# Delta-rule attention with two mixture layers on one core: the first group of linear systems on VectorE alone, P by partial sums, the second keys on ScalarE's queue

## What is computed

```
k_n = k / (|k| + 1e-6);  state = 0                       # 4 batches x 8 heads, 768 tokens, 48 features
for t: y_t   = q_t . state                               # with the state before the token
       state += beta_t * outer(k_n_t, v_t - state^T k_n_t)
x = y as 3072 tokens x 384
x = ((x@w1) * (x@w2)) @ w3 @ w_out                       # 384 -> 1024 -> 1024 -> 384
logits = x @ phi                                         # 32 slots
slots  = softmax(logits over tokens)^T @ x -> 8 experts of 4 slots: relu(s@e1)@e2
out    = softmax(logits over slots) @ slot_out
```

## Time and profile before

| | us |
|---|---|
| runs shown, lowest / median / highest | 546.17 / 548.49 / 549.38 |
| profiled execution: device time | 547.8 |
| profiled execution: span of the trace | 546.1 |
| PE busy | 495.9 (91%) |
| DVE / POOL / ACT busy | 249.7 / 207.8 / 139.0 |
| mean granted TensorE clock | 0.957 of full speed |

### The profile page before, as it was taken

One profiled execution on the slowest core, in us unless ns is written; L12 is line 12 of the kernel. 1 busy time (PEld: TensorE's weight loads), 2 busy tenths in 40 slices (PEclk: granted clock), 3 DMA queues, 4 the chain that ended last, 5 costly groups with the idle time before them and its releaser, 6 DMA issues.

```text
span 546.1 us, 24802 instructions
## 1 busy us (share of the span) xinstructions
PE 495.9 (91%) x11482; PEld 356.9 (65%) x11482; DVE 249.7 (46%) x537; ACT 139.0 (25%) x271; POOL 207.8 (38%) x386
## 2 busy tenths in 40 slices
PE   5797599979999999999899989999989999779974
PEld 5734457767777777777677867777767777324533
DVE  2699777255532554325462343633422421444424
ACT  0104212213222223222322223232212222104313
POOL 1077359850588006880048810488200000000000
PEclk9999589989999999999999999999999999689997
DMA  8996000440002500025000260000430607995938
GB/s 214 364 289 266 2 4 4 109 127 6 4 2 83 156 4 4 4 64 173 4 4 4 59 178 4 4 4 4 167 145 4 233 5 258 413 368 194 361 143 346
DMA packets 28439, 65.18 MB, mean 119 GB/s; under 512 B 1968, under 2 KB 15408, under 8 KB 28080
## 3 DMA queue, kind: packets, MB, share of 16 engines
q1 hardware_dynamic: 27888, 62.81, 34.2%
q10 hardware_dynamic: 448, 0.79, 0.6%
HBM read 58.87 MB, written 4.72 MB: 116 GB/s over the span
## 4 chain that ended last, share of the span: by engine, by line
PE 81%; DVE 9%; issue 4%; DMA 2%; ACT 1%; DVEq 0%
PE pB L1062 19%; PE pA L1062 18%; PE pD L1007 4%; PE pY L1017 4%; PE pK L989 4%; PE pK L967 3%; PE pT L1078 3%; PE pG L1078 3%; PE pY L974 2%; DVE prep_slab L673 2%; PE pD L1086 2%; DVE prep_slab L672 2%; PE pG L948 2%; PE pT L948 2%; PE pT L1028 2%
## 5 line engine op out<-in xcount | busy, mean ns | idle before, releaser
L428 POOL TENSOR_TENSOR prod_p<-prep_slab 128x84 f32<-128x84 f32 (+14 forms) x175 | 85.6, 489 | 49.3 <-DVE prep_slab L664 36.4
L429 POOL TENSOR_TENSOR prep_slab<-prep_slab,prod_p 128x84 f32<-128x84 f32 (+14 forms) x175 | 92.2, 527 | 13.7
L612 DVE TENSOR_TENSOR arena<-a_sb,pB 128x512 f32<-128x512 f32 x42 | 28.9, 688 | 142.7 <-PE pB L1062 142.5
L1062 PE MATMUL pB<-whi,xhi 128*128 128x512 f32 x138 | 59.6, 432 | 0.0
L1062 PE MATMUL pB<-whi,xlo 128*128 128x512 f32 x138 | 54.8, 397 | 0.4 <-issue 0.4
L1062 PE MATMUL pB<-wlo,xhi 128*128 128x512 f32 x138 | 54.5, 395 | 0.0
L1062 PE MATMUL pA<-whi,xhi 128*128 128x512 f32 x138 | 52.3, 434 | 0.0
L420 POOL TENSOR_SCALAR_AFFINE_SELECT prep_slab<-prep_slab 128x1024 f32<-128x1024 f32 x6 | 7.6, 1265 | 111.3 <-DVE sys_s L632 111.3
L1062 PE MATMUL pA<-whi,xlo 128*128 128x512 f32 x138 | 48.6, 402 | 0.0
L1062 PE MATMUL pA<-wlo,xhi 128*128 128x512 f32 x138 | 47.9, 400 | 0.8 <-issue 0.8
L471 ACT ACTIVATE a_sb<-pA 128x512 f32<-128x512 f32 x48 | 28.8, 600 | 68.8 <-PE pA L1062 61.0
(11 more groups left out here) (229 smaller groups left out, 844.3 us busy)
## 6 DMA issues: line engine op xcount, KB each, us to landing
late_w<-e_dram SPq DMA_DIRECT2D x8, 1536.0 KB, 9.1
arena<-kq_dram SPq DMA_DIRECT2D x44, 192.0 KB, 5.0
arena<-e_dram SPq DMA_DIRECT2D x5, 1536.0 KB, 11.7
arena<-kv_dram SPq DMA_DIRECT2D x16, 384.0 KB, 5.7
out_dram<-late_w SPq DMA_DIRECT2D x6, 768.0 KB, 5.3
arena<-w3t_dram SPq DMA_DIRECT2D x2, 2048.0 KB, 20.1
arena<-w_dram SPq DMA_DIRECT2D x1, 4096.0 KB, 14.1
late_w<-w_dram SPq DMA_DIRECT2D x2, 1536.0 KB, 19.7
```

Source lines behind the costliest of these rows:

```text
L428: link(nc.gpsimd.tensor_tensor(pv, a, x, ALU.mult))
L429: link(nc.gpsimd.tensor_tensor(dst, dst, pv, ALU.add))
L612: nc.vector.tensor_tensor(ab_tile(s, p)[:, half * HF:(half + 1) * HF], a_sb[:], pB[:], ALU.mult).then_inc(ab_done, 1)
L1062: last = mm((pA, pB)[w][:], lhs[:, c * 128:(c + 1) * 128], rhs[:, w, c, fc], start=(k == 0), stop=(k == 3 * KC - 1))
```

## The change

1. PE: `FILLERS` 80 -> 48.
2. Group 0 is solved by DVE alone, all columns in `X`, with no second copy in `At` and no mask by POOL: the mask comes with `first_keys`, which copies the Gram to `Gs` on DVE through `upto`. ACT copies the raw query-key part (`pt_raw`), and DVE masks it later in place (`first_pt`).
3. Step 0: R is values times norms (DVE, ahead of `scale`); `key_query_state` is left out; `y_step` goes ahead of `state_step` and starts the bank itself. In step 1 `up(0,0,0)` goes ahead of `key_query_state`, and the other parts change places.
4. P: the products of w_out and phi, and of wp and w3^T, go to separate 32-partition quadrants of a bank as partial sums; ACT copies them to `parts` and PE adds them by a product with `same`.
5. The second keys are issued from ACT's queue behind the copy of `wp`; kv of group 0 goes ahead of w1 on SP.
6. PE: after the Grams of group 1, 15 products of 128 x 512 (`AWAKE`), the one of k waiting for elimination step k of DVE, k = 15 to 29.
7. ACT: the Grams of group 1 are copied out before step 0, `w_high(0)` after them, `w_high(1)` in step 1.

```diff
-COL0_FIRST = 5
-FILLERS = 80
+FILLERS = 48
+AWAKE = range(15, 30)
 ...
-            reload_kq(1, 1)
+            load_kv(0, 0)
             sp.dma_start(w_raw[0], ...)
-            load_kv(0, 0)
             sp.dma_start(w_raw[1], ...)
-            sp.wait_ge(wp_ps, 1)
+            sp.wait_ge(part_ps, 2)
             load_kv(1, 1)
 ...  # POOL
+                if is_first(n):
+                    pool.wait_ge(x_link, 2)
+                    values(1, STEPS)
+                    return
 ...  # ACT
             for s in range(STEPS):
-                gram_out(0, s, first_gram[0][s])
+                act.wait_ge(gs_done, s + 1)
+                nc.scalar.activation(PT[0][:, s], <query-key part of the bank>, ACT.Copy).then_inc(pt_raw, 1)
+            part_out(0, 32 * KC)
+            part_out(1, 32 * KC)
             act.wait_ge(wp_ps, 1)
             nc.scalar.activation(wp_sb, pK[:, 0:FC * NS], ACT.Copy).then_inc(wp_done, 1)
-            pt_out(0)
-            w_high(0)
-            pt_out(1)
+            for i in range(H // 2):
+                for r in range(2):
+                    act.dma_start(*kq_piece(1, 1, i, r)).then_inc(kq_in[1][r], 16)
+            part_out(2, 128)
+            part_out(3, 128)
             act.wait_ge(p_ps, 1)
             nc.scalar.activation(P_sb, pY[:, 0:FC * NS], ACT.Copy).then_inc(p_done, 1)
-            w_high(1)
+            for s in range(STEPS):
+                gram_out(1, s, first_gram[1][s])
+            w_high(0)
 ...  # DVE
+            def first_keys(s, bank):
+                dve.wait_ge(gram_done, s + 1)
+                nc.vector.tensor_tensor(Gs[...s...], bank[... 0:C], upto[...], ALU.mult).then_inc(gs_done, 1)
 ...
-                for dst in (X, At) if is_first(n) else (X,):
-                    link(nc.vector.tensor_tensor(dst[:], At[:], ...
+                link(nc.vector.tensor_tensor(X[:], At[:], ...
 ...  # solve_first
-                    pv, a, x, dst = update(prod_d, At, k_, 0, min(k_, COL0_FIRST))
+                    pv, a, x, dst = update(prod_p, X, k_, 0, k_)
 ...
             solve_first()
+            r_rows(0, 0, 0, 0)
             scale(0)
             turn_back(0, 0)
                     if g == 0:
-                        r_rows(g, p, s, n)
+                        first_pt(0, 1)
                         for i in range(STEPS):
                             mask_pt(1, q, i, first_gram[1][i])
+                        first_pt(1, STEPS)
                         state(g)
                         set_up(1, q, k)
 ...  # PE
+            def add_parts(ps, rows_, sem_):
+                for c in range(FC):
+                    last = mm(ps[:, c * NS:(c + 1) * NS], parts[0:rows_, c * 128:(c + 1) * 128],
+                              same[0:rows_, 0:NS], start=True, stop=True)
+            for i in range(2):
                 for c in range(KC):
-                    last = mm(pK[:, g * NS:(g + 1) * NS], wot_raw[:, c, g * 128:...], phi_sb[:, c, :], ...)
+                    last = mm((pY, pK)[i][32 * c:32 * c + 32, :], phi_sb[:, c, :], wot_raw[:, c, i * HF:...], ...)
+            add_parts(pK, 32 * KC, wp_ps)
 ...
                 for c in range(FC):
-                    last = mm((pY, pK)[i][0:NS, :], wp_sb[:, c, :], w3t_raw[i][:, c, :], ...)
+                    g = c % 4
+                    last = mm((pY, pK)[i][32 * g:32 * g + 32, :], wp_sb[:, c, :], w3t_raw[i][:, c, :], ...)
+            add_parts(pY, 128, p_ps)
 ...
             for s in range(STEPS):
                 gram_products(1, s, first_gram[1][s])
+            for k_ in AWAKE:
+                pe.wait_ge(prep_link, X_LINK + 2 * k_)
+                mm(pK[:], ident[:], Macc[:, 0:HF], start=True, stop=True)
 ...
                     if g == 0:
                         solve_rows(g, p, s, n)
+                        y_step(g, p, s)
                         state_step(g, p, k, s, n)
-                        y_step(g, p, s)
                         x_turn(g)
                         continue
+                    if g == 1:
+                        up(t, 0, 0); key_query_state(g, p, k, s); up(t, 0, 1); solve_rows(g, p, s, n)
+                        up(t, 1, 0); state_step(...); ab_turn(...); y_step(g, p, s); up(t, 1, 1); x_turn(g)
+                        continue
```

More of the change, by code:

```diff
@@ L209, in delta_moe_kernel @@
         consts = sem("consts")
+        mask_in = sem("mask_in")
         diag_z = sem("diag_z")
@@ L422, in prep @@
                 pool.wait_ge(prep_link, prep_base(n) + X_LINK)
-                col0 = COL0_FIRST if is_first(n) else 0
-                for k_ in range(col0 + 1, C - 1):
-                    if not is_first(n) and k_ == VALUES_AT:
+                for k_ in range(1, C - 1):
+                    if k_ == VALUES_AT:
                         values(0, 1)
-                    pv, a, x, dst = update(prod_p, X, k_, col0, k_)
+                    pv, a, x, dst = update(prod_p, X, k_, 0, k_)
                     link(nc.gpsimd.tensor_tensor(pv, a, x, ALU.mult))
                     link(nc.gpsimd.tensor_tensor(dst, dst, pv, ALU.add))
-                if is_first(n):
-                    pool.wait_ge(x_link, 2)
-                    values(0, 1)
                 values(1, STEPS)
@@ L778, in _ @@
                                         ALU.add).then_inc(macc_done, 1)
-            for s in range(STEPS - 1):
-                mask_pt(0, 0, s, first_gram[0][s])
+            dve.wait_ge(macc_done, INIT_MACC)
+            nc.vector.tensor_tensor(upto[:], upper[:], same[:, 0:C], ALU.add).then_inc(mask_in, 1)
+            dve.wait_ge(mask_in, 1)
+            for s in range(STEPS):
+                first_keys(s, first_gram[0][s])
             set_up(0, 0, 0)
-            mask_pt(0, 0, STEPS - 1, first_gram[0][STEPS - 1])
             set_up_root(0)
@@ L954, in key_query_state @@
             def key_query_state(g, p, k, s):
-                if s == 0 and g > 0:
+                if s == 0:
                     for r in range(2):
@@ L1017, in y_step @@
                         last = mm(pY[o:o + 32, h * D:h * D + D], PT[p][q, s, h, :], Z[q, h, :],
-                                  start=False, stop=(h == H - 1), skip_group_check=True)
+                                  start=(g == 0 and h == 0), stop=(h == H - 1), skip_group_check=True)
                 last.then_inc(y_ps, 1)
@@ L1129, in _ @@
                     gram_products(0, s, first_gram[0][s], 2 * i, 2 * i + 2)
+            def add_parts(ps, rows_, sem_):
+                for c in range(FC):
+                    last = mm(ps[:, c * NS:(c + 1) * NS], parts[0:rows_, c * 128:(c + 1) * 128], same[0:rows_, 0:NS],
+                              start=True, stop=True)
+                last.then_inc(sem_, 1)
             pe.wait_ge(phi_in, 16)
             pe.wait_ge(wot_in, 16)
-            for g in range(FC):
+            for i in range(2):
                 for c in range(KC):
-                    last = mm(pK[:, g * NS:(g + 1) * NS], wot_raw[:, c, g * 128:(g + 1) * 128], phi_sb[:, c, :],
-                              start=(c == 0), stop=(c == KC - 1))
-            last.then_inc(wp_ps, 1)
+                    last = mm((pY, pK)[i][32 * c:32 * c + 32, :], phi_sb[:, c, :], wot_raw[:, c, i * HF:(i + 1) * HF],
+                              start=True, stop=True)
+                last.then_inc(part_ps, 1)
+            pe.wait_ge(macc_done, INIT_MACC)
+            pe.wait_ge(part_done, 2)
+            add_parts(pK, 32 * KC, wp_ps)
             pe.wait_ge(wp_done, 1)
@@ L1141, in _ @@
                 for c in range(FC):
-                    last = mm((pY, pK)[i][0:NS, :], wp_sb[:, c, :], w3t_raw[i][:, c, :], start=(c == 0),
-                              stop=(c == FC - 1))
-                last.then_inc(pt_ps, 1)
-            pe.wait_ge(pt_done, 2)
-            for c in range(FC):
-                last = nc.tensor.transpose(pY[:, c * NS:(c + 1) * NS], pt_sb[:, c * 128:(c + 1) * 128],
-                                           ident[0:NS, 0:NS])
-            last.then_inc(p_ps, 1)
+                    g = c % 4
+                    last = mm((pY, pK)[i][32 * g:32 * g + 32, :], wp_sb[:, c, :], w3t_raw[i][:, c, :], start=(c < 4),
+                              stop=(c >= 4), skip_group_check=True)
+                last.then_inc(part_ps, 1)
+            pe.wait_ge(part_done, 4)
+            add_parts(pY, 128, p_ps)
             pe.wait_ge(gs_done, STEPS)
-            pe.wait_ge(pt_mask, STEPS)
+            pe.wait_ge(pt_raw, STEPS)
             for r in range(2):
```

100 lines of the change are left out of this document (66 added, 34 removed).

## The result

The changed kernel takes 555.9 us (median of 4 runs, 553.8 to 557.2) against 547.3 for the kernel before (median of 4, one run more than the three shown above): a ratio of 1.016 with a 95% interval of [1.009, 1.024], so some 8 to 9 us slower.

| us | before | after | difference | forecast |
|---|---|---|---|---|
| start to step 0 | 59.5 | 70.0 | +10.4 | +0.7 |
| step 0 to step 4 | 64.4 | 65.5 | +1.1 | +1.2 |
| step 4 to step 23 | 319.7 | 317.6 | -2.1 | } +1.0 |
| step 23 to the end | 102.4 | 101.2 | -1.2 | |
| span | 546.1 | 554.3 | +8.2 | +2.9 |

The account below looks back on a forecast made before the run. PE was 91% busy, held until 59.54 us by group 0's preparation, mostly DVE. Terms 0.7 - 1.2 + 2.4 + 1.0 = +2.9 on 547.8 gave 550.7, forecast as a median of 551, range 541 to 557.

Parts of the forecast that it names:

- likeliest case: The forecast's own case: step 0 starts at 57.5 to 63 us, total 548 to 553.5 us; chance 0.43.
- third rival: Second keys on their own queue take turns with larger packets, landing at 46 us: 556.9 us, slower; chance 0.15.
- DVE's side: Ahead of step 0: Grams and copy, set-up and elimination shrink, sum -8.6 us, letting step 0 start at about 51.
- The second keys: Ahead of group 1's Grams: the keys on ACT's queue land at 39 us, bounds 31.6 to 46.
- half of the bytes: Second keys' share of transfers beside other traffic: 14.3 us for 1.57 MB, landing at 38.8 us.
- The Grams of group 1: Behind P and the second keys: 8.1 us with one wait for a code block, ending at 47.1 us.
- The 15 products: Behind group 1's Grams: 12.9 us back to back, 47.1 to 60.0, so step 0 at 60.2, +0.7 us.
- P: PE's chain ahead of step 0: products, copies and adding finish P at 36 us.
- POOL's start: Step 0 to step 4: POOL starts 13.2 us behind step 0, not 14.4, -1.2 us.
- The clock after the wait at step 4: Behind PE's wait at step 4: half clock on the path costs +2.4 us, bounds 0 and +4.
- Code blocks later: From step 4 on: shifted code-block boundaries lengthen gaps from 6.3 to 7.3 us, +1.0, bounds -2 and +4.
- first rival: Group 1's Grams end by 37 us, products wait for DVE, step 0 at 51: 542.6 us, faster; chance 0.27.

Follow-up runs that it names:

- x2: The changed kernel with the second keys issued by SP again, behind w3^T and ahead of kv: 545.4 us, ratio 0.996 to the kernel before.
- z1: The changed kernel with SP issuing kv of both groups, w1 and w2 only once the second keys, on ACT's queue, have landed: 547.1 us, one run.
- x1: The changed kernel without its 15 added products ahead of step 0: 557.2 us, ratio 1.015 to the kernel before.
- y1: The kernel before with 48 fillers instead of 80, nothing else changed: 555.0 us, ratio 1.015 to the kernel before.
- w3: Changed kernel, second keys on SP, group 1's set-up in step 0 behind the state's update, 15 products 32x32, 64 fillers instead of 48: 541.3 us, ratio 0.986.
- x4: The changed kernel with the second keys on SP's queue and the 15 added products made 32x32: 539.5 us, ratio 0.989 to the kernel before.
- v3: Changed kernel, second keys on SP, group 1's DVE set-up in step 0 around the state's update, only the last 5 added products: 543.0 us, ratio 0.993.

## Why the prediction was right in its range and wrong in its step

The value, 551, has the wrong mechanism behind it. The measured 555.9 lies outside the likeliest case's own range (548 to 553.5) and inside 541 to 557 only because that range reached into the rivals. It is the third rival's case (late keys, 556.9), which was given 0.15, and part of that rival's closeness is luck too: it had the start of step 0 at +6.9 us and the rest at +2.2, and the spans show +10.4 and -2.2. Its turns also gave the keys one byte to five or eight of the other queue, and the trace has one to 2.4.

- **DVE's side: right.** Transpose -2.1 (forecast -2.0), set-up 7.3 us from the transpose on (9.9 less 2.7 is 7.2), elimination 22.0 (22.4), TM at 50.4, start allowed at 51. One size was off: the masking copy takes 0.59 us, not 0.42. The row that it was sized from reads a mask and a bank as well (L638 still takes 0.42 here); the new one writes `Gs` in another order of elements, and whether that is the reason no run shows.
- **The second keys: wrong.** "I take 39"; they landed at 50.7, outside the bounds of 31.6 to 46. The 39 is the sum's value for "half of the bytes", and that share had no row behind it: while both queues had work, the keys got 85 GB/s of 290, under a third, and the total was below the bulk's own 409 as well. x2 and z1 show this step alone to be the loss: the Grams start at 36.8 and 36.7 with it mended.
- **The Grams of group 1: 6.0 us, not 8.1.** It has no gap for code in it: the packet for the block in question begins at 52.4, 3.1 us before PE comes to that place. In x2 the gap is there (2.42; the packet begins at 40.9, PE goes on at 43.5) and the Grams take 9.0.
- **The 15 products: right.** 13.1 us (12.9), back to back, none waiting for DVE. But 13 us there aren't 13 us at the end: x1 gives all of it back.
- **P: right enough and hidden.** Its copy starts at 34.5 (36 forecast).
- **POOL's start: right.** 13.4 us behind step 0 (13.2).
- **The clock after the wait at step 4: right.** From the end of `xlo` to `solve_rows` of step 4 it is 5.6 us instead of 3.5, +2.1 (+2.4).
- **Code blocks later: wrong sign.** -2.1 up to step 23 and -1.2 behind it, not +1.0; the gaps between 130 and 455 us went from 9.9 to 8.3. This hid 4 us of the keys' error and put the forecast nearer to the result than it deserved. Of the 3.3 us the gaps between 130 and 455 us account for 1.6; where the rest comes from is not shown.

With the measured terms the sum is 10.4 - 0.9 + 2.1 - 3.3 = +8.3; the spans differ by 8.2.

Had the keys landed at 39 as forecast, x2 shows what comes: step 0 at 59.5 (forecast 60.2), +1.2 to step 4 (+1.2), then -1.4 and -1.5 for the code where I had +1.0; span -1.8, median 545.4 and not 551. So two steps failed, with opposite signs: the landing of the keys by 10 us of start, the code places by 4 us. The first rival (products done in time) couldn't come with the keys mended either: PE ends its work on P at 34.5 to 36.7 in the changed kernel, x2 and z1, and even with 6.0 us the Grams behind it end past 40, and not by the 38 from which it decides (45.8 in x2).

## What to carry to other kernels

Transfers that the next step waits for go ahead of bulk transfers on the same queue, not on a queue of their own beside them. An earlier start is worth only what the next join lets through: look for what sets that (here POOL's start, which a move of 8 us of DVE work advanced by 12 us) before shortening the way to it. And where one engine issues thousands of small instructions, compare variants at an equal count: here 40 to 128 records more or less, at places that cost next to nothing, went with 8 to 10 us, so a gain of 1% from an edit that changes the count cannot be credited to the edit.

## What the runs showed of the hardware

- Between 130 and 455 us PE's gaps for code stand at 193 modulo 256 records in all thirteen traces, 0.6 to 3.9 us each, 7 to 15 us in sum. The Trainium skill, Runtime: NRT & Kernel Launch, section Instruction fetch mechanics, has blocks of 256 instructions fetched ahead; the spacing agrees, and so do the packets of the instruction queue, 16,384 bytes for every 256 records. Each gap ends 2.2 to 3.0 us after the start of such a packet, and with the count the places shift, as y1 and w3 show; x4, with the changed kernel's count, has most of its gaps at the changed kernel's places.
- 192 KB pieces on a queue of their own land every 2.4 us beside bulk rows, and without them all eight land 5.1 to 6.1 us after their issue. The two queues moved equal numbers of packets (721 and 724 from 31 to 46 us), and the sum of both is below the bulk's own rate (286 against 409 GB/s).
- How much the sum of the gaps changes with a shift could not be forecast, and four tries missed: the prediction (+1.0 us, measured -3.3), y1 (at most +4 behind step 4, measured +6.8), v3 (3 us either way, the time 8 us off) and w3 (2 us less of gaps, measured 2 us more). What decides it stays open; so does how much of the 7 to 12 us between step 4 and step 23 is the gaps and how much the half clock that goes with them (3.4 to 13.8 us in the stretch of the table).
